# Cross and read products of a linear-attention kernel: from one masked 128-column product per pair of heads to four 64x64 products

## What is computed

```
for t in range(S):
    y[:, :, t] = einsum('bhd,bhde->bhe', rt, state)
    Sa = einsum('bhde,bhe->bhd', state, at)
    state = state * wt[:, :, None, :] - einsum('bhd,bhe->bhde', Sa, bt) + einsum('bhd,bhe->bhde', vt, kt)
...
x = attn_out as (B * S, H * D)
h = (x @ w1) * (x @ w2) @ w3 @ w_out
h = maximum(h @ w_in, 0);  out = (h * h) @ w_out2
```

## Time and profile before

| | us |
|---|---|
| median of 3 runs (range) | 1058.69 (1058.61 to 1059.34) |
| the profiled execution's own time | 1060.74 |
| its span, first to last instruction | 1059.0 |
| PE busy | 1023.2 (97%) |
| DVE, POOL, ACT busy | 634.7, 486.1, 419.7 |

### The profile page before, as it was taken

One profiled execution on the slowest core, in us unless ns is written; L12 is line 12 of the kernel. 1 busy time (PEld: TensorE's weight loads), 2 busy tenths in 40 slices (PEclk: granted clock), 3 DMA queues, 4 the chain that ended last, 5 costly groups with the idle time before them and its releaser, 6 DMA issues.

```text
span 1059.0 us, 27606 instructions
## 1 busy us (share of the span) xinstructions
PE 1023.2 (97%) x11008; PEld 880.8 (83%) x11008; DVE 634.7 (60%) x1005; ACT 419.7 (40%) x796; POOL 486.1 (46%) x1573
## 2 busy tenths in 40 slices
PE   5998989999999999999999999999999999999998
PEld 5786768779898888898888898888988888897797
DVE  6876366777875656666567566467567555442333
ACT  3453434454543343443344343334434234332332
POOL 4777755527447346346346355355365364200000
PEclk8997999999999999999999999999999999999999
DMA  9953556756886764757665757756648744555552
GB/s 177 188 127 65 155 132 170 197 165 203 226 234 178 170 150 126 180 145 180 151 157 131 176 140 202 150 134 155 160 125 217 154 117 132 154 169 184 166 170 75
DMA packets 267390, 169.05 MB, mean 160 GB/s; under 512 B 199680, under 2 KB 229376, under 8 KB 267264
## 3 DMA queue, kind: packets, MB, share of 16 engines
q1 hardware_dynamic: 267264, 167.29, 62.7%
HBM read 141.03 MB, written 26.21 MB: 158 GB/s over the span
## 4 chain that ended last, share of the span: by engine, by line
PE 79%; DVE 4%; ACT 2%; issue 1%; ACTq 0%; DVEq 0%
PE aside L866 31%; PE moe_bank L953 16%; PE moe_bank L938 8%; PE both L830 3%; PE both L730 3%; PE both L768 3%; PE both L840 2%; PE both L844 2%; PE both L760 2%; PE both L811 2%; PE both L743 1%; PE both L819 1%; PE both L793 1%; PE both L853 1%; PE both L716 1%
## 5 line engine op out<-in xcount | busy, mean ns | idle before, releaser
L671 POOL TENSOR_TENSOR inv_tmp<-blk,inv 128x60 f32<-128x60 f32 (+24 forms) x744 | 209.5, 282 | 358.4 <-DVE blk L1480 301.4
L675 POOL TENSOR_TENSOR inv<-inv,inv_tmp 128x60 f32<-128x60 f32 (+24 forms) x744 | 237.4, 319 | 58.3
L953 PE MATMUL moe_bank<-v_ring,h_hi 128*128 128x320 f32 x768 | 175.3, 315 | 0.0
L866 PE MATMUL aside<-x2T_hi,w_ring 128*128 128x512 f32 x480 | 148.0, 405 | 4.4 <-DVE h_lo L1548 4.3
L866 PE MATMUL aside<-xT_hi,w_ring 128*128 128x512 f32 x480 | 148.2, 406 | 2.2 <-DVE h_lo L1548 1.5
L1558 DVE SCALAR_TENSOR_TENSOR aside<-aside,left 128x512 f32<-128x512 f32 x96 | 66.9, 697 | 122.0 <-ACT left L1258 122.0
L953 PEld LDWEIGHTS moe_bank<-v_ring,h_hi 128*128 128x128 f32 x768 | 128.0, 188 | 3.9
L1548 DVE TENSOR_TENSOR h_lo<-aside,h_hi 128x512 fp32r<-128x512 f32 x144 | 97.4, 677 | 49.7 <-ACT h_hi L1250 49.0
L1250 ACT CAST h_hi<-aside 128x512 fp32r<-128x512 f32 x144 | 84.7, 588 | 94.9 <-DVE aside L1558 49.6
L953 PE MATMUL moe_bank<-v_ring,h_lo 128*128 128x320 f32 x384 | 118.6, 309 | 0.0
L1258 ACT ACTIVATE left<-aside 128x512 f32<-128x512 f32 x96 | 57.4, 598 | 117.3 <-PE aside L866 117.3
(11 more groups left out here) (151 smaller groups left out, 1604.2 us busy)
## 6 DMA issues: line engine op xcount, KB each, us to landing
w_ring<-gate_rows SPq DMA_DIRECT2D x40, 640.0 KB, 4.6
w_ring<-win_rows SPq DMA_DIRECT2D x40, 640.0 KB, 4.1
v_ring<-wout_rows SPq DMA_DIRECT2D x80, 320.0 KB, 3.1
v_ring<-fold_rows SPq DMA_DIRECT2D x48, 320.0 KB, 4.2
gate_rows<-w_ring SPq DMA_DIRECT2D x8, 640.0 KB, 6.4
win_rows<-w_ring SPq DMA_DIRECT2D x8, 640.0 KB, 4.4
wout_rows<-v_ring SPq DMA_DIRECT2D x16, 320.0 KB, 5.9
stage<-in_moe_w SPq DMA_DIRECT2D x8, 512.0 KB
```

What stands on the lines that cost most here:

```text
L671: nc.gpsimd.tensor_tensor(tmp, x[:, j, 0:j].unsqueeze(2).broadcast_to([P, j, X - lo]), mine[:, j:j + 1, lo:X].broadcast_to([P, j, X - lo]) ...
L675: nc.gpsimd.tensor_tensor(mine[:, 0:j, lo:X], mine[:, 0:j, lo:X], tmp, ALU.add).then_inc(solve, 1)
L866: last = nc.tensor.matmul(bank(use), w, x, start=n == 0, stop=n == len(terms) - 1)
L953: last = nc.tensor.matmul(bank(f"o{s}")[:, 0:M], h[at % RING][:, s * P:(s + 1) * P], weights[:, rest * M:(rest + 1) * M], start=f == 0 and ...
```

## The change

Cross and read become 32 products each instead of 8: for each pair, both halves of the weights (z) against both heads (q), with the 40 rows of that head alone, 64 weight columns and 64 moving columns. The output's partition half is z, and head q's results lie in bank q. The two heads' tiles no longer share columns of a product, so `azk` needs no zeros: the first clearing of both `azk` buffers, `reset` on ACT and `clear` on POOL go, and `scale_a` waits for the `make_z` that last read the buffer instead. `mask_ak`, `copy_blocks`, and `make_y` read the results from their new places, and `ruv` is stored by head, then pair. Nothing else moves.

```diff
+        def of_head(n, q, rows=slice(0, P)):
+
+            return (its_first, its_second)[q](n)[rows].rearrange("s (x t) -> s x t", x=X)
...
-        clears = [azk[0], rbd[0], azk[1], rbd[1], *spare, *zv, *sT, *st]
+        clears = [*rbd, *spare, *zv, *sT, *st]
...
-            def clear(n):
-                at = 2 * (n - OPENING)
-                pool.wait_ge(z_made, n + 1)
-                pool.wait_ge(solve, (STEPS + 1) * (n + 1))
-                wait(pool, azk_cleared, at)
-                nc.gpsimd.memset(azk[n % 2][DP:P, :, 0, :], 0.0).then_inc(azk_cleared, 1)
-                pool.wait_ge(azk_cleared, at + 1)
-                nc.gpsimd.memset(azk[n % 2][0:DP, :, 1, :], 0.0).then_inc(azk_cleared, 1)
...
-                wait(pool, azk_cleared, 2 * (n - OPENING))
...
             def cross(n):
                 pe.wait_ge(scaled_bk, n + 1)
                 for x in range(X):
-                    last = nc.tensor.matmul(its_both(n)[:, x * P:(x + 1) * P], bkT[n % 2][0:E, x].rearrange("e z s -> e (z s)"),
-                                            azk[n % 2][0:E, x].rearrange("e q t -> e (q t)"), start=True, stop=True)
+                    for z in range(2):
+                        for q in range(2):
+                            rows = half_rows(q, D)
+                            last = nc.tensor.matmul(of_head(n, q, half_rows(z))[:, x], bkT[n % 2][rows, x, z, :],
+                                                    azk[n % 2][rows, x, q, :], start=True, stop=True)
                 last.then_inc(crossed, 1)
...
                 for x in range(X):
-                    last = nc.tensor.matmul(its_both(n)[:, x * P:(x + 1) * P], uvT[0:E, x, :],
-                                            rbd_of(n)[0:E, x].rearrange("e q t -> e (q t)"), start=True, stop=True)
+                    for z in range(2):
+                        for q in range(2):
+                            rows = half_rows(q, D)
+                            last = nc.tensor.matmul(of_head(n, q, half_rows(z))[:, x], uvT[rows, x, half_rows(z)],
+                                                    rbd_of(n)[rows, x, q, :], start=True, stop=True)
                 last.then_inc(read_made, 1)
...
-            def reset(n):
-                act.wait_ge(z_made, n + 1)
-                for q in range(2):
-                    rows = half_rows(1 - q)
-                    nc.scalar.copy(azk[n % 2][rows, :, q, :], zeros[rows].unsqueeze(1).broadcast_to([DP, X, C])).then_inc(
-                        azk_reset, 1)
...
-                if n < 2:
-                    dve.wait_ge(cleared, 2 * n + 1)
-                elif n < OPENING + 2:
-                    dve.wait_ge(azk_reset, 2 * (n - 1))
-                else:
-                    dve.wait_ge(azk_cleared, 2 * (n - 1 - OPENING))
+                wait(dve, z_made, n - 1)
...
-                    nc.vector.tensor_copy(diag[rows], by_pair(n, rows)[:, :, 1, BLK * at:BLK * (at + 1)])
+                    nc.vector.tensor_copy(diag[rows], of_head(n, 1, rows)[:, :, BLK * at:BLK * (at + 1)])
...
-                    nc.vector.tensor_tensor(azk[n % 2][rows, :, q, :], by_pair(n, rows)[:, :, q, :],
+                    nc.vector.tensor_tensor(azk[n % 2][rows, :, q, :], of_head(n, q, rows),
```

More of the change, by code:

```diff
@@ L138, in attention_with_experts @@
         uvT = sb("uvT", [P, X, 2 * C])
-        ruv = sb("ruv", [P, X, 2, C])
+        ruv = sb("ruv", [P, 2, X, C])
         state_tmp = sb("state_tmp", [P, X, D])
@@ L190, in attention_with_experts @@
             sem("u1_copied"), sem("uvT_copied"), sem("state_placed"), sem("st_copied"))
-        solve, azk_cleared, azk_reset = sem("solve"), sem("azk_cleared"), sem("azk_reset")
+        solve = sem("solve")
         y_stored = [sem(f"y_stored{h}") for h in range(2)]
@@ L676, in invert @@
                     at += 2
-            for n in range(OPENING + 1):
+            for n in range(WINDOWS):
                 invert(n)
-            for n in range(OPENING, WINDOWS):
-                clear(n)
-                if n + 1 < WINDOWS:
-                    invert(n + 1)
         @block.tensor
@@ L844, in make_y @@
                         last = nc.tensor.matmul(its_first(n)[half_rows(q, D), x * C:(x + 1) * C], bk_row[half][:, x, q, :],
-                                                ruv[:, x, q, :], start=False, stop=True, skip_group_check=True)
+                                                ruv[:, q, x, :], start=False, stop=True, skip_group_check=True)
                 last.then_inc(y_made, 1)
@@ L1165, in copy_r @@
                 if n < OPENING:
-                    act.wait_ge(cleared, (2, 4, 5, 6)[n])
+                    act.wait_ge(cleared, n + 1)
                 else:
@@ L1177, in copy_blocks @@
                     rows = slice(BLK * at, BLK * (at + 1))
-                    nc.scalar.copy(diag[rows], by_pair(n, rows)[:, :, 0, BLK * at:BLK * (at + 1)])
+                    nc.scalar.copy(diag[rows], of_head(n, 0, rows)[:, :, BLK * at:BLK * (at + 1)])
                 for q in range(2):
@@ L1181, in copy_blocks @@
                     wait(act, masked_ak, (2 * n + 1) * q)
-                    nc.scalar.copy(n10[n % 4][lo:lo + BLK], by_pair(n, slice(lo, lo + BLK))[:, :, q, BLK:C]).then_inc(
+                    nc.scalar.copy(n10[n % 4][lo:lo + BLK], of_head(n, q, slice(lo, lo + BLK))[:, :, BLK:C]).then_inc(
                         blocks_copied, 1)
@@ L1331, in _ @@
             copy_x(0)
-            reset(0)
             copy_r(1)
@@ L1338, in _ @@
             copy_x(1)
-            reset(1)
             copy_r(2)
@@ L1359, in _ @@
             copy_x(2)
-            reset(2)
             copy_u(1, 1, u1_made, u1_copied)
@@ L1370, in _ @@
             copy_x(3)
-            reset(3)
             copy_u(2, 1, u1_made, u1_copied)
@@ L1513, in mask_read @@
                 dve.wait_ge(read_made, n + 1)
-                nc.vector.tensor_tensor(ruv[:].rearrange("s x q t -> s (x q) t"),
+                nc.vector.tensor_tensor(ruv[:].rearrange("s q x t -> s (q x) t"),
                                         its_both(n).rearrange("s (y t) -> s y t", t=C),
```

## The result

| | us |
|---|---|
| before, median of 6 runs (range) | 1058.76 (1055.99 to 1062.16) |
| after, median of 6 runs (range) | 1040.44 (1037.36 to 1042.99) |
| ratio, 95% interval | 0.9823 (0.9803 to 0.9843) |
| the profiled execution of after, its span | 1040.6, 1038.9 |

The changed kernel is 18.3 us faster; 1039.3 was forecast.

The account below looks back on a forecast made before the run. TensorE, busy 97% of the span, was taken to bound the loop: -19.8 us for 38 groups, -0.6 for the opening and +1 given back make -19.4, so the median 1058.69 would become 1039.3; range 1032 to 1063.

Parts of the forecast that it names:

- The group: Each cross or read on TensorE, as 16 rounds of four passes, was to cost 1.27 us against 1.79, gaining 0.52.
- L760's pace: Existing TensorE row with 64 weight and 40 moving columns, 60 ns a pair of passes; taken as the new round's length.
- L768 as the nearest row: TensorE products on two diagonal quarters overlap, 22 ns a record; taken to show that products sharing columns overlap too.
- The sum: Whole kernel: 19.8 us from 38 loop groups and 0.6 from the opening, less 1 given back: 19.4 us faster.
- The opening: Before the loop, only the shorter first cross counts: 2.79 to 2.0 us, about 0.6 gained, all inversions starting earlier.
- The foretold risk: A TensorE stall in the opening could move the lower-clock stretch to where TensorE is the bound; no size given.
- What is given back: Shorter groups cover less DVE and ACT expert work, so TensorE's loop waits could grow by 1 us, at most some 4.
- The clearings: Removing POOL's memsets and ACT's copies was to gain nothing; for ACT's copies at most their 4.9 us.
- Rival 1: In the groups, products on the same columns run in turn, a loss of 0.44 us each: 1070 to 1078, chance 0.15.
- Rival 2: Instruction issue limits the groups at 20 ns a record, gain only 0.23 us each: 1045 to 1052, chance 0.15.
- Rival 3: A floor of 25 ns for each matmul makes a group 1.88 us, a loss of 0.09: 1062, chance 0.04.
- Rival 4: Groups get shorter but the loop's waits take the gain back: 1051 to 1058 us, chance 0.06.

Follow-up runs that it names:

- e5_after: The changed kernel run again, unchanged, as the measure for the runs beside it: 1042.37 us, ratio 0.9825.
- e6_clears: The changed kernel with all clearings of the azk buffers and their waits put back: 1041.05 us, ratio 0.9819.
- e10_resets: The changed kernel with only ACT's clearing copies in the opening put back: 1040.99 us.
- e11_pool: The changed kernel with only POOL's clearings put back, its memsets and the first two: 1039.26 us.
- e7_read_only: The kernel before with only the read changed to the new products; old cross and the clearings it needs kept: 1049.61 us, ratio 0.9906.
- e2_runs: The changed kernel with four products in a row on each quarter in the cross, eight in the read: 1124.42 us.
- e1_order: The changed kernel with the cross alternating output halves first and the read doing two products in a row on each quarter: 1042.47 us.
- e12_swap: The changed kernel with ACT's copy of u moved ahead of the rounding of an expert slice, in iteration 7 only: 1040.26 us.

## Why the prediction was right, point by point

**The group.** The working held almost to the nanosecond for what it rested on: four at once, L760's pace for 64 weight columns, and the extra costs on the way in and out. A round takes 58 ns, between the 56 and 60 of the two rows, and the first takes 107, 49 more, which the 0.03 "for the first round" had somewhat low. 0.52 a group was forecast and 0.507 is what 30 groups of the settled loop give. The choice of L768 as the nearest row for products on the same columns, against the row of "in turn", decided the sign, and it was right. L819, L760 and L768 kept their lengths.

**The sum.** The span fell by 20.1: 3.3 up to `turn_inverse(5)`, 1.1 to inverse 8, 15.2 to inverse 23, 0.5 behind it. Forecast were 19.8 for 38 groups, 0.6 for the opening and 1 given back. One of the 38 groups, the read of window 4, lies ahead of `turn_inverse(5)`. So the groups brought 19.3, what is given back is 1.9 (6 groups brought 1.1 for 3.0), twice the 1 of the forecast, and the opening gave 2.8 for 0.6. The mechanism was right; these two errors went opposite ways, and that the forecast time is within 1.1 us of the measured median is in part luck. PE's waits, 8.1 us, were also just over the "under 8 us" that the prediction had named as its sign (7.1 in e5_after).

**The opening.** POOL's first inversion started at 21.35 us, where 22.5 was forecast, and PE's timeline says why. After:

```profile
14.45 1.16 PE L723 MATMUL both<-azk,bkT 40*64 40x64 f32 x64
15.54 0.65 PE L690 MATMUL aside<-ident,w_raw 64*104 64x64 f32 x8
```

e6_clears:

```profile
14.62 1.85 PE L737 MATMUL both<-azk,bkT 40*64 40x64 f32 x64
16.40 0.37 PE L704 MATMUL aside<-ident,w_raw 64*104 64x64 f32 x3
```

In after the first cross already runs at its later pace, 1.09 us. In e6_clears most of it runs slowly, as in the earlier trace rows, and it takes 1.78 for the 2.79 of before; the inversion started at 22.2. So the change is worth 1.0 us there. The forecast had 2.0 for this cross, 1.6 times the 1.27 that includes the ways in and out, where the 2.79 is from start to next start; 1.07 by 1.6 would have been 1.7. And 2.79 less 2.0 is 0.8, not the 0.6 that went into the sum. "At the lower clock" was read from the pace. The view gives 1.00 for 14.54:16.40 us of before as for 16.40:17.33, but the trace's first clock record starts only at 16.4 us, and the records of the cross start 213 ns apart before that and 111 behind it. The pace rises at another time in each execution: the same new cross takes 1.09 in after and e10_resets, 1.34 in e5_after, 1.56 in e11_pool and 1.78 in e6_clears, and the old one 2.45 in e7_read_only, whose first inversion started 0.55 us earlier than before with nothing changed ahead of it. Of the other 0.8 us of after 0.7 are this quicker pace of the first cross. What of the remaining 1.5 of the 3.3 belongs to the change, beside the 0.5 of the one group, isn't settled: up to `turn_inverse(5)` the short-group kernels took 174.7 to 178.3 us against 179.35, and the read alone 180.7, so single executions differ there by more than the term. That the ten groups of the opening "give nothing by themselves" may be too strong: DVE came 1.7 us late for `turn_inverse(4)` before and not after, though no run separates the groups from the place of the slow stretches there. The foretold risk, a stretch at half clock that moves to where PE is the bound, did come (140.7 to 150.9 us), and the stretch up to `turn_inverse(5)` was 3.3 us shorter all the same.

**What is given back.** The waits of the loop grew by 2.3 us (1.3 in e5_after), more than the 1 that was taken and within the bound of 4, but by another way than foretold. The prediction said that PE waits never for a DMA. It doesn't directly; it did so through ACT's order, and the row `PE both L811 <- issue` in the earlier trace rows was the place. "Issue" there meant only that the view named no releaser.

**The clearings** cost nothing end to end, as forecast, and the masks too: L1471's successor L1451 has the same 689 ns as in the earlier trace rows, so reading 512 in a row instead of alternating blocks brought nothing.

**The rivals.** Rival 1 (products on shared columns in turn) fell to the slice with four records and to the group's 1.09 us. Rival 2 gave 20 ns a record; the group has 58 ns for four. Its other half, a queue that can't look far ahead, is real (e2_runs), but the order of the change asks every quarter in turn and never meets it. Rival 3: a floor of 25 ns would have made 1.88 us of the group's 1.29. The Trainium skill, "TensorE: Matmul & The Clock Gate", section "Wait — 56ns, not 53.3ns?", states it for starts of matmuls; here four records start within 35 ns and the 64 starts of a read lie within 0.94 us, 15 ns in the mean, so it doesn't hold across quarters. Within one quarter they are 58 ns apart, so nothing here speaks against it there. Rival 4 took 1.9 us.

## What to carry to other kernels

Small products that share no quarter of the array run four at once even when two of them write to the same columns, if the program asks the quarters in turn: one or two products a quarter, not four or eight. These products had the two heads' results in different banks; one bank for both was not tried. Size such a group by its rounds (58 ns for 64 by 64 in float32 passes) plus some 0.36 us for the way in and out (1.29 less 16 rounds), and don't stop at halves: half-array tiles were slower than the full one here. And where the profile gives "issue" as a wait of the bounding engine, look up what the engine that feeds it is waiting for; a full DMA system can stand behind it.

## What the runs showed of the hardware that I had not expected

- The waiting line of a quarter. 1.09, 1.24, 2.62 and 3.33 us for the same products in runs of 1, 2, 4 and 8; the theory of one running and two waiting passes foretold two further orders to 0.01 us. The theory is tested on these shapes only, and products of two heads in one bank, the layout before, were not tried as quarters.
- The granted clock fell behind slow groups. e2_runs lost 82 us against e1_order, but its groups explain 69.5 (18 crosses by 1.53, 20 reads by 2.10). In its loop the granted clock falls nine times for 3.4 us, each time within 0.5 us of the end of one of these groups, in which mostly one quarter is at work for 2.6 to 3.3 us; in e1_order, after and the other kernels with 1.09 or 1.24 us groups it doesn't fall there. From inverse 8 to 23, with seven of the nine, e2_runs took 65.0 us more than e1_order where the groups make 54.4, so some 1.5 us for each fall. Not every slow group is followed by one, and what decides it isn't shown. The columns of this view of e2_runs are those of the earlier trace rows:

```profile
255.00:260.30 5.30, 5.30 (x74) 4.65 (x73) 2.42 (x6) 2.60 (x6) 4.28 (x14) 1.00 0.87 276
260.30:263.70 3.40, 3.40 (x20) 3.07 (x20) 2.03 (x3) 0.00 (x0) 2.70 (x10) 0.50 0.38 79
```

  PE counts as busy all the time, and yet the granted clock is 0.50, the 1.2 GHz level, in the second window.
- The loop itself is exact to 0.1 us from execution to execution (590.0 us for inverse 8 to 23 in six kernels, e12_swap among them); nearly all of the spread of the end times arises ahead of 305 us, where the stretches at half clock lie differently in each execution.
